# Attention with top-1 routing on one core: row products on halves of the array, and batch 0's work issued ahead of batch 1's pack scores

## The reference, cut to what matters

```python
p_packed = sm_attn(p, k, v)            # [b, h, 32, 64]
out = sm_attn(q, p_packed, p_packed)   # [b, h, 576, 64]
x = out.transpose(0, 2, 1, 3).reshape(4608, 512)
logits = normalized(x) @ normalized(expert_emb).T / tau
expert_idx = argmax(logits)            # one of 8 experts a token
x = gate_w * (relu(x @ w1[e]) @ w2[e])
out = (h * sigmoid(h)) @ w_out         # h = x @ w_in
```

## Time and profile before

| what | value |
|---|---|
| median of 3 runs | 1456.26 us (1453.97 to 1456.88) |
| the profiled execution's own time | 1453.96 us |
| its span, first to last instruction | 1452.2 us |
| instructions | 27808 |
| mean granted TensorE clock | 0.993 |
| TensorE busy in the span | 97% |
| VectorE, ScalarE, POOL busy | 68%, 34%, 39% |
| mean DMA rate over the span | 160 GB/s |

### The profile page before, as it was taken

How to read it: one execution, slowest core, us unless ns; L and a number is a source line. 1 busy time by engine, 2 the same in 40 slices (tenths; PEclk the granted TensorE clock), 3 DMA queues, 4 the chain that set the end, 5 groups by cost and what they waited for, 6 DMA issues and landing times. The chain is left out here.

```text
span 1452.2 us, 27808 instructions
## 1 busy us (share of the span) xinstructions
PE 1414.0 (97%) x9813; PEld 1274.6 (88%) x9814; DVE 982.0 (68%) x1382; ACT 493.9 (34%) x749; POOL 565.8 (39%) x466
## 2 busy tenths in 40 slices
PE   7999999999999999999999999999999999999996
PEld 4676688778888888888999999999989999999996
DVE  4888554444444444446888888888898778777783
ACT  3887400330001120203554444444453333333331
POOL 1466708797702870705753333332250111101111
PEclk9999999999999999999999999999999999999998
DMA  9994745786513651514444443443683343333430
GB/s 341 356 355 142 274 131 142 219 267 168 205 48 101 210 201 67 169 43 175 133 139 136 121 125 118 128 130 117 204 265 131 117 144 128 132 130 116 144 116 29
DMA packets 141911, 232.99 MB, mean 160 GB/s; under 512 B 11544, under 2 KB 94872, under 8 KB 134304
## 3 DMA queue, kind: packets, MB, share of 16 engines
q1 hardware_dynamic: 103984, 145.24, 30.4%
q10 hardware_dynamic: 26736, 58.65, 12.2%
q0 software_dynamic: 11136, 28.40, 5.8%
HBM read 144.86 MB, written 87.38 MB: 160 GB/s over the span
## 5 line engine op out<-in xcount | busy, mean ns | idle before, releaser
L792 PE MATMUL ps<-wf,xf 128*128 128x256 f32 x3024 | 365.1, 284 | 4.8 <-DVE xf L1912 4.0
L792 PEld LDWEIGHTS ps<-wf,xf 128*128 128x128 f32 x3024 | 364.5, 193 | 5.4 <-DVE xf L1912 2.8
L792 PE MATMUL ps<-xf,wf 128*128 128x256 f32 x2646 | 323.8, 284 | 0.1
L792 PEld LDWEIGHTS ps<-xf,wf 128*128 128x128 f32 x2646 | 319.1, 192 | 0.3 <-ACT cb L1319 0.3
L792 PE MATMUL ps<-weights,hT 128*128 (+1 forms) x1032 | 246.5, 394 | 0.8 <-DVE hT L1798 0.8
L792 PE MATMUL ps<-weights,xT 128*128 (+1 forms) x1008 | 242.0, 395 | 2.4 <-POOL weights L2054 2.0
L792 PEld LDWEIGHTS ps<-weights,hT 128*128 128x128 f32 x1032 | 190.4, 188 | 39.7 <-issue 1.1
L792 PEld LDWEIGHTS ps<-weights,xT 128*128 128x128 f32 x1008 | 185.7, 188 | 41.4 <-issue 4.5
L1185 ACT CAST weights<-stage 128x1024 fp32r<-128x1024 f32 x56 | 58.0, 1052 | 383.4 <-PE ps L792 284.6
L2054 POOL TENSOR_TENSOR weights<-stage,weights 128x1024 fp32r<-128x1024 f32 x56 | 132.6, 2405 | 132.1 <-ACT weights L1185 132.1
L2201 POOL TENSOR_TENSOR h<-h,sg 128x512 f32<-128x512 f32 x72 | 100.3, 1394 | 188.3 <-ACT sg L1333 188.1
(11 more groups left out here) (233 smaller groups left out, 1755.7 us busy)
## 6 DMA issues: line engine op xcount, KB each, us to landing
g_rows<-h SPq DMA_DIRECT2D x144, 256.0 KB, 2.6
raw<-g_rows SPq DMA_DIRECT2D x36, 1024.0 KB, 4.8
stage<-w ACTq DMA_DIRECT2D x53, 512.0 KB, 3.8
w_forms<-fm ACTq DMA_DIRECT2D x16, 896.0 KB
x_in<-x_rows SPq DMA_DIRECT2D x43, 256.0 KB
y_rows<-y_sb SPq DMA_DIRECT2D x43, 256.0 KB
wf_f<-w_forms SPq DMA_DIRECT2D x11, 896.0 KB, 5.2
q_sb<-qT SPq DMA_DIRECT2D x8, 1152.0 KB
```

The lines of the kernel that those rows point to most:

```text
L792: mm = pe.matmul(o, left(a_), right(b_), start=first and n == 0, stop=last and n == 2)
```

## The change

**Row products.** `rhs` becomes 272 columns wide: 8 logit columns, 256 of the heads, 8 logit columns, in both groups. `keep_pl` writes the logits of packs in partitions 0 to 63 on the left and those in 64 to 127 on the right, in four copies instead of two; the other halves of those columns are not read. A row product becomes six matmuls that contract over 64 partitions each, by turns over the upper half (partitions 0 to 63, to one bank) and the lower half (64 to 127, to the other bank): 136 columns each of group 0 upper and group 1 lower, 8 columns each that add the other group's logits, and 128 columns each of the other group. Each skips the columns that are zero in its half. The upper half's bank now holds the first pairs of heads of both groups and the lower half's bank the second pairs, so x has its four 128-column chunks in the order 0, 2, 1, 3; the table STORED undoes it where the experts' first matmul takes its chunks. For the last tile of 64 tokens a bf16 matmul of one element comes first.

**The start.** Batch 0's second value product goes to bank 6 (`value_bank`), so it needs no wait for the first. On TensorE, both value products, both turns and both token-score products of batch 0 come ahead of batch 1's first pack scores; three pairs of `stay_warm` matmuls are taken out and one pair is put ahead of the second token scores. ScalarE and VectorE follow: both `keep_ppt`, both `exp_tokens` of batch 0, both `diagonal`, `turn_scores` and `top_tokens` are moved out of `batch(0)` or ahead, and the diagonals stand ahead of the waits for tau.

```diff
@@ -44,7 +44,8 @@
 NG = H // 4
-XW = 4 * D + E
+XW = 4 * D + 2 * E
+XB = 4 * D + E
 KD, KF, KF2 = DM // P, F // P, F2 // P
@@ -81,6 +82,7 @@
 X_AT = (0, 1, 6, 5, 2, 3, 4)
+STORED = (0, 2, 1, 3)
 G_AT = (1, 2, 6, 0, 3, 4, 5)
@@ -361,17 +363,17 @@
+        def value_bank(b, g):
+            return bank[6] if isinstance(b, int) and b == 0 and g == 1 else bank[3]
         def rank_bank(b):
...
-            return rhs[par][g][:, E:XW] if g == 0 else rhs[par][g][:, 0:4 * D]
-        def packs_lg(par, g):
-            return rhs[par][g][:, 0:E] if g == 0 else rhs[par][g][:, 4 * D:XW]
+            return rhs[par][g][:, E:E + 4 * D]
@@ -601,20 +603,20 @@
                     pe.wait_ge(v_in[par], 32 * (r + 1))
-                if not (isinstance(G, int) and G == 0):
+                if not (isinstance(b, int) and b == 0):
                     pe.wait_ge(ppt_kept, G)
...
                         lo = g * 4 * D + j * P
-                        mm = pe.matmul(bank[3][64 * j:64 * j + 64, 0:P], pk_eT[g][:, c, 64 * j:64 * j + 64],
+                        mm = pe.matmul(value_bank(b, g)[64 * j:64 * j + 64, 0:P], pk_eT[g][:, c, 64 * j:64 * j + 64],
                                        v_sb[par][:, c, lo:lo + P], start=c == 0, stop=c == TPB - 1)
...
                 for j in range(2):
-                    mm = pe.transpose(bank[3][:, 4 * D + j * P:4 * D + (j + 1) * P],
+                    mm = pe.transpose(value_bank(b, g)[:, 4 * D + j * P:4 * D + (j + 1) * P],
                                       own(par, g)[:, j * P:(j + 1) * P], ident)
@@ -654,9 +656,20 @@
                 lo = row_bank(b, k)
-                for g in range(NG):
-                    mm = pe.matmul(bank[lo + g][0:m, 0:XW], tk_aT[g][:, k * P:k * P + m], rhs[par][g],
-                                   start=True, stop=True)
+                if m < P:
+                    pe.matmul(bank[lo][0:1, XB:XB + 1], ones[:, 0:1], ones[:, 0:1], start=True, stop=True)
+                token = slice(k * P, k * P + m)
+                up_, dn = slice(0, 64), slice(64, P)
+                left, mid, end = slice(0, E), slice(E, E + 2 * D), slice(E + 2 * D, XB)
+                own_0, own_1, lg_1 = slice(0, E + 2 * D), slice(E + 2 * D, XW), slice(XB, XW)
+                for rows, o, at, g, cols, first_, last_ in (
+                        (up_, bank[lo], slice(0, E + 2 * D), 0, own_0, True, False),
+                        (dn, bank[lo + 1], slice(2 * D, XB), 1, own_1, True, False),
+                        (up_, bank[lo], left, 1, left, False, True),
+                        (dn, bank[lo + 1], slice(4 * D, XB), 0, lg_1, False, True),
+                        (up_, bank[lo], end, 1, mid, True, True),
+                        (dn, bank[lo + 1], slice(0, 2 * D), 0, slice(E + 2 * D, XB), True, True)):
+                    mm = pe.matmul(o[0:m, at], tk_aT[g][rows, token], rhs[par][g][rows, cols], start=first_, stop=last_)
                 mm.then_inc(x_done, 1)
@@ -684,10 +697,12 @@
                     rows_tokens(b - 1, other, 0, False)
-                turn_values(b, par, 1)
+                if not first:
+                    turn_values(b, par, 1)
                 if not last:
                     scores_packs(b + 1, rn, other, 1)
-                scores_tokens(b, r, par, 1, False)
+                if not first:
+                    scores_tokens(b, r, par, 1, False)
                 if first or last:
@@ -739,21 +754,21 @@
             turn_packs(0, 1)
-            stay_warm(2, o=5)
             pe.wait_ge(pad_rows, 1)
             values_packs(0, 0, 0, 0)
-            stay_warm(2, o=5)
+            values_packs(0, 0, 0, 1)
             pe.wait_ge(init_done, 1)
             turn_values(0, 0, 0)
-            values_packs(0, 0, 0, 1)
-            stay_warm(2, o=5)
+            turn_values(0, 0, 1)
+            scores_tokens(0, 0, 0, 0, True)
             pe.wait_ge(en_step, 3)
...
             mm.then_inc(en_step, 1)
+            stay_warm(2)
+            scores_tokens(0, 0, 0, 1, True)
             scores_packs(1, 0, 1, 0)
-            scores_tokens(0, 0, 0, 0, True)
             pe.wait_ge(en_step, 5)
@@ -808,7 +823,7 @@
                         lo = c * F + n * 512
-                        mm = three(bank[n], lambda a_: xT[:, a_, c, :], lambda b_: w[:, b_, lo:lo + 512],
+                        mm = three(bank[n], lambda a_: xT[:, a_, STORED[c], :], lambda b_: w[:, b_, lo:lo + 512],
                                    c == 0, c == KD - 1)
@@ -867,7 +882,7 @@
                     lo = c * F + n * 512
-                    mm = three(bank[n], lambda a_: x[:, a_, c, :], lambda b_: w[:, b_, lo:lo + 512], c == 0, c == KD - 1)
+                    mm = three(bank[n], lambda a_: x[:, a_, STORED[c], :], lambda b_: w[:, b_, lo:lo + 512], c == 0, c == KD - 1)
                     yield mm
@@ -1055,12 +1070,15 @@
                 act.copy(ppT[par][:, 2 * g:2 * g + 2, :].rearrange("p j k -> p (j k)"),
-                         bank[3][:, 4 * D:8 * D]).then_inc(ppt_kept, 1)
+                         value_bank(b, g)[:, 4 * D:8 * D]).then_inc(ppt_kept, 1)
...
                 act.wait_ge(pl_done, b + 1)
-                act.copy(packs_lg(par, 0), bank[2][:, 0:E])
-                act.copy(packs_lg(par, 1), bank[2][:, E:2 * E]).then_inc(pl_kept, 1)
+                for g in range(NG):
+                    lg = bank[2][:, g * E:(g + 1) * E]
+                    act.copy(rhs[par][g][0:64, 0:E], lg[0:64])
+                    kept = act.copy(rhs[par][g][64:P, XB:XW], lg[64:P])
+                kept.then_inc(pl_kept, 1)
@@ -1078,7 +1096,7 @@
                 act.copy(x_row[par][0:m, k, :].rearrange("p (g c) -> p g c", g=NG),
-                         ps[0:m, lo:lo + 2, 0:XW]).then_inc(x_kept, 1)
+                         ps[0:m, lo:lo + 2, 0:XB]).then_inc(x_kept, 1)
@@ -1099,7 +1117,8 @@
                     first_hi(b, r, par)
-                keep_ppt(b, par, 1, first or fresh)
+                if not first:
+                    keep_ppt(b, par, 1, fresh)
                 if not first:
@@ -1108,12 +1127,13 @@
                 keep_pl(b, par)
-                exp_tokens(b, 0)
                 if not first:
+                    exp_tokens(b, 0)
                     keep_x(b - 1, rn, other, 2, fresh)
...
                     keep_turn(b + 1, 0, False)
-                exp_tokens(b, 1)
+                if not first:
+                    exp_tokens(b, 1)
                 if first:
@@ -1138,7 +1158,10 @@
             keep_ppt(0, 0, 0, True)
+            keep_ppt(0, 0, 1, True)
+            exp_tokens(0, 0)
             exp_packs(1, 0, False)
+            exp_tokens(0, 1)
             batch(0, 0, 0, first=True)
@@ -1473,7 +1496,7 @@
                     dve.wait_ge(x_done, TPB * (b - 1))
-                pairs = bank[3][:, 0:P].rearrange("p (o n) -> p o n", o=1).to_broadcast([P, 2, P])
+                pairs = value_bank(b, g)[:, 0:P].rearrange("p (o n) -> p o n", o=1).to_broadcast([P, 2, P])
                 dve.scalar_tensor_tensor(own(par, g).rearrange("p (o n) -> p o n", o=2), pairs, pk_inv[:, g:g + 1],
@@ -1585,9 +1608,10 @@
                     max_packs(b + 1, 1)
-                top_tokens(b, 0)
-                turn_scores(b, 1)
-                top_tokens(b, 1)
+                if not first:
+                    top_tokens(b, 0)
+                    turn_scores(b, 1)
+                    top_tokens(b, 1)
                 sum_tokens(b, 0)
@@ -1611,9 +1635,11 @@
             dve.tensor_copy(upper, cs[:, C_UP:C_UP + P]).then_inc(init_done, 1)
+            dve.wait_ge(init_done, 1)
+            diagonal(0, 0, 0, True)
+            diagonal(0, 0, 1, True)
             dve.wait_ge(tau_in, 16)
             dve.reciprocal(itau[:, 1:2], itau[:, 0:1]).then_inc(tau_done, 1)
-            dve.wait_ge(init_done, 1)
             dve.wait_ge(tau_done, 1)
@@ -1622,13 +1648,14 @@
             dve.tensor_scalar(emb_n, emb_n, en[:, 3:4], itau[0:E, 1:2], ALU.mult, ALU.mult).then_inc(en_step, 1)
-            diagonal(0, 0, 0, True)
-            diagonal(0, 0, 1, True)
+            turn_scores(0, 0)
+            top_tokens(0, 0)
             dve.wait_ge(en_step, 4)
...
             dve.tensor_copy(embT.rearrange("p c e -> p (c e)"), bank[7][:, 0:KD * E]).then_inc(en_step, 1)
+            turn_scores(0, 1)
+            top_tokens(0, 1)
             max_packs(1, 0)
-            turn_scores(0, 0)
             batch(0, 0, 0, first=True, fresh=True)
```

## The result

The changed kernel takes **1460.94 us** (median of 8 runs, 1456.87 to 1465.33), the kernel before 1453.62 (8 runs on the same chip, 1451.32 to 1456.88): ratio **1.0046**, 95% interval 1.0034 to 1.0058. It is slower by twice the 0.2% that the forecast took for what a measurement can tell. The forecast was 3.5 us faster, 1452.8, with a range up to 1458; the kernel is 7.3 us slower and the time lies outside the range. The profiled execution took 1462.32 us, span 1460.5.

What follows compares the result with a forecast made beforehand. TensorE was taken to set the pace, with the whole effect in the first 151.5 us. Batches -1.5, start -1.7 and end -0.3 sum to -3.5 us: 1452.8 from the median 1456.26, range 1445 to 1458.

Steps and rivals of the forecast that it cites:

- Row products: TensorE's row products: array halves overlap fully, 0.76 us each against 0.99; with switches, -0.11 us a batch.
- the switch between tilings: On TensorE, between matmuls of different array tiling: about 0.10 us each, with the load behind it exposed.
- Rivals 1: Row halves' weight loads don't overlap: 1.38 us a product instead of 0.76, total 1469 us; chance 10%.
- 2: Rival 2: row halves need no drain at tiling switches, a batch saves 1.35 us, total 1446 us; chance 15%.
- 3: Rival 3: row products take half their time, 2.5 us a batch less on TensorE, total 1445 us; chance 5%.
- the batch's -0.25 us: Each of batches 1 to 6: -0.11 from row products, -0.14 from product 3's shorter hold; -1.5 us in all.
- Rival 5: Batch held by transfers or copies: steady gain nil, total 1454.5 us; chance 6%.
- keep_pl: ScalarE's logit copies, four instead of two: two more at some 0.06 us, costing nothing, or 0.12 a batch uncovered.
- The stall of product 3: Product 3, held some 0.2 us by ScalarE's copy of product 2, starts sooner as product 2 ends earlier: -0.14 us.
- The start: New issue order brings batch 2's pack scores (L581) from 33.62 to 31.9 us: -1.7, bounds -3.0 and +0.6.
- rival 4: Clock falls again at the start as TensorE idles without fillers: start +0.6 instead of -1.7, total 1455 us; chance 17%.
- The end: Row products of batch 7, paced by ScalarE's copies: -0.3 us, bounds 0 and -1.

Runs made afterwards that it cites:

- e3: The changed kernel with keep_pl's four copies writing all 128 partitions instead of 64 each; 1457.76 us, ratio 1.0018 to the kernel before.
- e2: The kernel before with only the six half-array matmuls, their layout and the four copies, its start unchanged; 1461.91 us, ratio 1.0045 to the kernel before.
- e8: e1 with bf16 filler matmuls (2, 4 and 6) in three idle stretches of the start; 1452.41 us, ratio 0.9992 to the kernel before.
- e4: e3 with two filler matmuls ahead of row product 3 in each batch but the first and last; 1457.91 us, ratio 1.0017 to the kernel before.
- e9: e3 with e8's fillers at the start; 1459.30 us, ratio 1.0025 to the kernel before.
- e11: e9 with six more fillers in the last batch, ahead of product 2 and of its own first product; 1458.48 us, ratio 1.0014 to the kernel before.
- e10: The changed kernel, split copies kept, with e8's fillers at the start; 1460.28 us, ratio 1.0043 to the kernel before.
- e7: e3 with ScalarE's copy of row product 2 ahead of the first token-score exp; 1462.10 us, ratio 1.0069 to the kernel before.
- e5: The changed kernel with the six matmuls of every row product issued twice; 1475.55 us, ratio 1.0154 to the kernel before.
- e12: e8 with the second expert chunk's load issued behind batch 2's k and p; 1452.29 us, ratio 0.9981 to the kernel before.
- e1: The kernel before with only the changed kernel's order at the start; 1456.38 us, ratio 1.0003 to the kernel before.

## Why the prediction was wrong

**Row products, right.** Overlap of the halves, 0.88 us from start to start (0.76 + 0.10), 0.115 for a narrow pass (0.106), the switch between tilings. Rivals 1, 2 and 3 are out: they needed some 1.5, 0.76 and 0.5 us from start to start. By part, against the earlier trace rows, the batch's five products with their neighbours changed by +0.06, +0.02, -0.03, -0.21 and -0.07, together -0.23; the forecast had -0.11.

**The step that failed first: the batch's -0.25 us.** It was -0.11 of products and -0.14 of a shorter stall of product 3, and nothing for keep_pl. Measured: -0.23 and +0.35; the batch's length came out 0.10 over before's. The products did better than forecast, and the whole miss is the stall. Rival 5 (6%), a batch held by transfers or copies, named what happened: ScalarE's copy holds it.

**keep_pl, wrong.** The step was "two more at some 0.06 us of issue ... nothing", and 0.12 a batch if uncovered. The copies cost 0.70 us up to the exp where two had cost 0.12. The row of 0.06 was of copies on all partitions; copies on alternating halves were priced by it without a row of their own. And the cover was sought in the wrong place: the turn of packs was named as the one who waits, but the exp and the x_row copy are queued behind on the same engine. Its share of the stall is the smaller part: with the price gone in e3, the wait went from 0.51 to 0.39.

**The stall of product 3, wrong.** The forecast held it for a consequence of product 2's end and let it shrink by 0.14. For the kernel before the rows allow that reading (copy at 74.66, product 2 over at 74.62); but the chain on ScalarE, logits, keep_pl, exp, was over only 0.2 us earlier, at 74.42, and the forecast didn't ask what a longer one would do. In the changed kernel it is this chain that the copy stands behind, and from the last turn of packs to product 3 it takes 0.77 us (77.87 to 78.64) instead of 0.42. e3 takes the copies' price out and gets 15.28, still 0.20 above the forecast. Of the rest the rows show that the logits' group takes longer with a switch in front (1.10 us from its start to the copies instead of 0.99) and the 0.3 us in which ScalarE stands idle ahead of the copy; the latter is unexplained.

**The start, wrong, and right in its times by luck.** The -1.7 was the distance from a row of before taken with the clock low (33.62, behind 6.83 us at 1.2 GHz) to a new start reckoned at full clock, and was put down to the order. e2 shows the old order at full clock: batch 2's pack scores at 31.56 and the first product at 34.80, e8 with the new order 31.84 and 35.07. The order gives nothing that can be told; what there was to gain was the clock's. And the change, which took fillers out and left gaps of 1.22 and 2.29 us, lost that too: the start of rival 4 (17%) came true, +0.5 us against its +0.6, though not its total of 1455.

**The end, wrong.** Forecast -0.3, measured +1.7: 0.7 at full clock up to batch 7's first own product, and 1.0 over the low stretch behind it, for which the forecast had no term.

**The clock in the batches, missing.** No step and no rival held that a busy TensorE could lose its clock in a steady batch. It is the largest term: in the profile four falls of 1.5 us make some 6 of the 8.3 us of span, the longer one at the end up to 1.0, and over the runs the changed kernel has 33.6 us of low time where the sets of before have 15.7 to 17.6. e3, e4, e9 and e11, whose batches are as long as before's or shorter, still are 0.14 to 0.25% slower; the wait at the end of attention that e9 shows may be a part of that; how much over the runs isn't shown. The four falls, and e9's one in a batch, begin 0.4 to 0.6 us behind the start of product 3 with the gap ahead of it, but the two undisturbed batches have the same gap, so the gap alone doesn't decide. Four falls in the batches are much for one execution: the profiles of e2, e9, e10 and e11 have one, those of e3, e4 and e7 none. Steadier is a fall around the end of attention, beginning between 144 and 154 us: it stands, 3.4 us or longer, in the profiles of all kernels with half-array products but e5, and in e12's, and not in those of before, e1 and e8. e5 shows that more work of the same kind removes the falls. What sets them off stays open: less work and more idle time are both there in the changed kernel, but e4, with the gap filled and TensorE busier than before, kept most of its low time, and e7, with more idle time still, shows no fall in a batch.

## What to carry to other kernels

Before shortening the work of an engine that sets the pace, follow what waits behind the next engine's queue: a product that takes 0.11 us less is worth nothing if the copy that the next product needs comes later. Compare a new order with a row of the old one at the same clock; here the whole forecast gain of the start lay between a slow row and a fast one. Where TensorE's clock has been at its upper level through a loop, count a change of that loop as a risk, and read the low time of several executions, not of one, before and after. Price an instruction by a row of the same partitions, not only of the same size.

## What the runs showed of the hardware that was not expected

- ScalarE: 8-column copies from PSUM on 128 partitions start 0.06 us apart; on alternating halves of 64 partitions 0.17 to 0.18 apart, no overlap (e3 against the change).
- TensorE's granted clock went from 2.4 to 1.2 GHz in batches where TensorE was busy for 14.5 of 15.4 us; with its products doubled it did not.
- At the end of attention two engines went on some 4 us behind the recorded end of the matmul that they waited for, in six kernels, for about 2.6 us of time; the cause is unknown.
- Two row halves of the array, each with its own loads, overlap fully: six matmuls of 12 passes in 0.88 us from start to start, which is 0.78 without a switch of 0.10 (an estimate from the earlier trace rows), and a second set 0.68.
- One stretch of 3.41 us at the lower clock costs a batch 1.5 us. Where the falls come changes from execution to execution, and that makes the spread: 8.5 us over the changed kernel's 8 runs, 5.6 to 11.0 over the sets of before, 2.6 over e12's 12.
